# First group of a fused kernel: W2's pieces rounded one pair of matmuls later, pieces and decays dealt out anew between GpSimd and VectorE, first tile evicted by VectorE

## The reference

```python
for t in range(S):                                   # linear attention with decay w
    cur = einsum('bhd,bhe->bhde', u * kt, vt)
    y[:, :, t] = einsum('bhd,bhde->bhe', rt, state + cur)
    state = w * state + einsum('bhd,bhe->bhde', kt, vt)
x = y as rows of 384
xn = (x - mean) / sqrt(var + 1e-6) * g_ln            # channel mixing
x = x + relu(xn @ w_ch1) @ w_ch2                     # 384 -> 1536 -> 384
e = expert of the token (argmax of logits, or the one before, by a gate)
out = p[e] * (relu(x @ w1[e]) @ w2[e])               # 384 -> 1024 -> 384, 8 experts
```

## Time and profile before

| | us |
|---|---|
| time, median of 3 runs (lowest to highest) | 398.2 (398.12 to 398.61) |
| the profiled execution's own time | 399.55 |
| its span | 397.7 |
| PE busy | 382.9 (96%) |
| DVE busy | 229.1 (58%) |
| ACT busy | 161.8 (41%) |
| POOL busy | 121.8 (31%) |
| DMA moved | 54.90 MB, mean 138 GB/s |

### The profile page before, as it was taken

The page is one execution under the profiler, slowest core; times in us unless marked ns, Lnnn a source line. Parts: engine busy times, 40 slices in busy tenths (PEclk is TensorE's granted clock), DMA queues, the critical chain, the costliest instruction groups (busy, mean ns, idle before and its releaser), DMA issues.

```text
span 397.7 us, 8980 instructions
## 1 busy us (share of the span) xinstructions
PE 382.9 (96%) x3173; PEld 348.2 (88%) x3173; DVE 229.1 (58%) x463; ACT 161.8 (41%) x300; POOL 121.8 (31%) x112
## 2 busy tenths in 40 slices
PE   8796999999999999999999999999999999999993
PEld 6686999999999999999999955689999999999983
DVE  7867954622633462254376947888854665629351
ACT  5636223232322323232244145376745672555530
POOL 2893190650362054000000400622332233223232
PEclk9997999999999999999999999999999999999999
DMA  7995300520330042310105578399893559201111
GB/s 214 325 328 151 107 21 23 159 75 20 105 106 20 20 154 77 131 50 2 39 3 203 175 213 284 106 348 320 297 370 124 186 139 369 76 31 42 28 40 45
DMA packets 32633, 54.90 MB, mean 138 GB/s; under 512 B 3261, under 2 KB 20323, under 8 KB 32592
## 3 DMA queue, kind: packets, MB, share of 16 engines
q1 hardware_dynamic: 30288, 48.07, 37.1%
q0 software_dynamic: 2304, 6.30, 5.3%
HBM read 49.64 MB, written 5.51 MB: 139 GB/s over the span
## 4 chain that ended last, share of the span: by engine, by line
PE 91%; DMA 2%; ACT 2%; DVE 1%; issue 1%; SPq 1%; POOLq 0%; DVEq 0%
PE bank L1000 7%; PE bank L894 6%; PE bank L896 6%; PE bank L895 6%; PE bank L1002 6%; PE bank L1006 6%; PE bank L1299 5%; PE bank L1307 5%; PE bank L1271 5%; PE bank L1303 5%; PE bank L1278 5%; PE bank L1275 5%; PE bank L1288 3%; PE bank L909 3%; PE bank L1200 3%; PE bank L1177 3%
## 5 line engine op out<-in xcount | busy, mean ns | idle before, releaser
L687 ACT ACTIVATE parts<-bank 128x512 fp32r<-128x512 f32 x36 | 21.5, 596 | 75.6 <-PE bank L1006 75.6
L1462 DVE SCALAR_TENSOR_TENSOR parts<-bank,parts 128x512 fp32r<-128x512 f32 x36 | 24.9, 692 | 47.4 <-ACT parts L687 47.3
L630 POOL DMA_INDIRECT out_y<-late x14 | 20.5, 1462 | 93.7 <-DVE late L1805 93.7
L894 PE MATMUL bank<-parts 128*128 128x384 f32 x144 | 49.0, 341 | 0.0
L896 PE MATMUL bank<-parts 128*128 128x384 f32 x144 | 48.2, 335 | 0.0
L895 PE MATMUL bank<-parts 128*128 128x384 f32 x144 | 48.1, 334 | 0.0
L770 ACT ACTIVATE parts<-stage (+1 forms) x32 | 46.2, 1486 | 2.3 <-DMA stage<-in_w 2.2
L1000 PE MATMUL bank<-xnT_hi,parts 128*128 128x256 f32 x216 | 41.5, 301 | 3.2 <-DVE parts L1421 3.2
L1774 DVE TENSOR_TENSOR parts<-stage,parts x24 | 41.1, 1755 | 5.2 <-ACT parts L770 4.5
L1006 PE MATMUL bank<-xnT_lo,parts 128*128 128x256 f32 x216 | 38.2, 286 | 0.0
L1002 PE MATMUL bank<-xnT_hi,parts 128*128 128x256 f32 x216 | 38.2, 286 | 0.0
(11 more groups left out here) (245 smaller groups left out, 763.1 us busy)
## 6 DMA issues: line engine op xcount, KB each, us to landing
stage<-in_w SPq DMA_DIRECT2D x36, 768.0 KB, 7.8
stage<-in_w_ch SPq DMA_DIRECT2D x6, 768.0 KB, 10.1
arena<-in_k_t SPq DMA_DIRECT2D x12, 224.0 KB, 3.9
arena<-in_r_t SPq DMA_DIRECT2D x12, 224.0 KB, 3.1
arena<-in_v_rows SPq DMA_DIRECT2D x12, 192.0 KB, 4.2
arena<-in_k_rows SPq DMA_DIRECT2D x12, 192.0 KB, 3.6
x_rows<-stage SPq DMA_DIRECT2D x12, 192.0 KB, 1.9
arena<-in_r_rows SPq DMA_DIRECT2D x10, 192.0 KB, 3.3
```

What stands on the lines that cost most here:

```text
L687: act.activation(hT_hi[:, 2 * q:2 * q + 2, :].rearrange("p a t -> p (a t)"), bk[6 + q % 2][:], ACT.Relu).then_inc(h_hi_ready, 1)
L894: pe.matmul(out_, a_lo, b_hi, start=start, stop=False)
L1462: dve.scalar_tensor_tensor(hT_lo[:, at, :].rearrange("p a t -> p (a t)"), bk[6 + q % 2][:], 0.0, hT_hi[:, at, :].rearrange("p a t -> p (a ...
```

## The change

It touches the start and the first group only; nothing is added to or taken from the later groups and the experts.

- **ScalarE** rounds piece 3 behind pair 2's eviction (before: behind pair 1's), piece 4 behind pair 3's and the decay (before: behind pair 2's), piece 5 behind pair 4's. It rounds piece 0 in two halves, with the centring of the two tiles between them, it evicts only the second tile's transpose, and it makes `w_chunk` (before: VectorE).
- **VectorE** evicts the first tile's transpose alone (`first_turned`: hi, then lo), does the decays of chunk 2 (`third_decays`), masks half of chunk 0's scores before the decays of chunk 1, and `coefs(2)` behind `masked(2)`. It no longer makes lo of pieces 1 and 4, nor the product `rkT[1]`.
- **GpSimd** takes over these: `second_products`, lo of piece 1 behind both halves of piece 0, and lo of piece 4 behind `diagonal(3)`, once VectorE has made lo of pieces 2 and 3. It drops the decays of chunk 2.
- **TensorE** has ten small matmuls without use more (`keep_warm(5)`) ahead of the first transpose. Pair 2 waits for `lo_p` 3 (GpSimd's piece 1), step f = 4 for `lo_p` 4 (GpSimd's piece 4).
- **SP** issues piece 5 behind `lo_p` 3 (before: behind `lo_v` 1).

The diff, cut to its core:

```diff
-LO_V = 1, 2, 3, 4, 5
+LO_V = 2, 3, 5
@@ SP, piece(i)
                     if i == 4:
                         sp.wait_ge(lo_p, 2)
                     else:
-                        sp.wait_ge(lo_v, LO_V.index(i - 4) + 1)
+                        sp.wait_ge(lo_p, 3)
@@ GpSimd
+            def second_products():
+                pool.wait_ge(kdec_ready, 2)
+                pool.wait_ge(rdec_ready, 2)
+                pool.tensor_tensor(rkT[1], kT[1], rT[1], ALU.mult).then_inc(rkT_ready, 1)
+
+            def rest_of_piece(i):
+                pool.wait_ge(hi_done, i + 2)
+                pool.tensor_tensor(piece_at(i, 1), piece_stage(i), piece_at(i, 0).bitcast(F32),
+                                   ALU.subtract).then_inc(lo_p, 1)
...
             k_decays(1)
+            second_products()
             diagonal(0)
...
+            diagonal(1)
             ends(0)
-            diagonal(1)
             first_piece(0)
             ends(1)
             first_piece(1)
-            for c in (2, 3):
-                decays(c)
-                if c == 2:
-                    pool.wait_ge(lo_v, 1)
-                    pool.wait_ge(s_u, 16)
-                rows(c)
-                ends(c)
+            pool.wait_ge(kdec_ready, 3)
+            rest_of_piece(1)
+            pool.wait_ge(s_u, 16)
+            rows(2)
+            ends(2)
+            diagonal(2)
+            decays(3)
+            rows(3)
+            ends(3)
+            diagonal(3)
+            pool.wait_ge(lo_v, 2)
+            rest_of_piece(4)
+            pool.wait_ge(lo_v, len(LO_V))
@@ ScalarE, group(g)
                 hidden(g, range(1, 2))
-                if first:
-                    round_piece(3)
-                else:
+                if not first:
                     logits(g - 1, 1)
                 decay(g * 2 + 2, 0)
                 hidden(g, range(2, 3))
                 if first:
-                    round_piece(4)
+                    round_piece(3)
                 hidden(g, range(3, 4))
                 decay(g * 2 + 3, 1)
                 if first:
+                    round_piece(4)
+                hidden(g, range(4, 5))
+                if first:
                     round_piece(5)
-                hidden(g, range(4, NHP))
+                hidden(g, range(5, NHP))
@@ ScalarE, start
-            round_piece(0)
-            act.wait_ge(s_ng, 1)
+            act.activation(w_chunk[:], pw[:, :, C - 1], ACT.Copy).then_inc(s_wc, 1)
+            round_first(0)
             for u in range(2):
                 centre_tile(0, u)
-            for u in range(2):
-                turned_tile(0, u)
+            round_first(1)
+            act.wait_ge(s_ng, 1)
+            turned_tile(0, 1)
             round_piece(1)
@@ TensorE, hidden
-                        if q < 2:
+                        if q < 3:
                             pe.wait_ge(lo_p, q + 1)
-                        elif q % 2 == 0:
-                            pe.wait_ge(lo_v, LO_V.index(q // 2) + 1)
+                        elif q == 4:
+                            pe.wait_ge(lo_v, LO_V.index(2) + 1)
@@ TensorE, rows_out
-                        pe.wait_ge(lo_v, LO_V.index(KD + f // 4) + 1)
+                        pe.wait_ge(*((lo_p, 4) if f == 4 else (lo_v, LO_V.index(KD + f // 4) + 1)))
@@ TensorE, start
+            keep_warm(5)
             pe.wait_ge(coef_ready, 2)
             turn_tile(0, 0)
@@ VectorE
+            def third_decays():
+                dve.wait_ge(s_turned[0], T_FIRST[0] + T_LOADS)
+                dve.tensor_tensor(rT[0], rT[0], w_r, ALU.mult).then_inc(rdec_ready, 1)
+                dve.tensor_tensor(kT[0], kT[0], w_k, ALU.mult).then_inc(kdec_ready, 1)
...
-            dve.tensor_copy(w_chunk[:], pw[:, :, C - 1]).then_inc(s_scan, 1)
-            dve.wait_ge(s_ng, 1)
-            turned(0)
-            rest_of_piece(1)
+            first_turned()
+            turned(0, range(1, 2))
+            third_decays()
```

More of the change, by code:

```diff
@@ L556, in diagonal @@
                                    coef[u][:].unsqueeze(2).to_broadcast([P, H, D]), ALU.mult).then_inc(cv_ready, 1)
+            def second_products():
[6 more added lines that the diff above has]
+                                   ALU.subtract).then_inc(lo_p, 1)
             def first_piece(half):
-                pool.wait_ge(hi_done, 1)
+                pool.wait_ge(hi_done, half + 1)
                 at = slice(half * GT, (half + 1) * GT)
@@ L579, in _ @@
             first_piece(1)
-            for c in (2, 3):
-                decays(c)
-                if c == 2:
-                    pool.wait_ge(lo_v, 1)
-                    pool.wait_ge(s_u, 16)
-                rows(c)
-                ends(c)
+            pool.wait_ge(kdec_ready, 3)
[11 more added lines that the diff above has]
+            pool.wait_ge(lo_v, len(LO_V))
             for g in range(NG - 1):
-                diagonal(2 * g + 2)
-                diagonal(2 * g + 3)
-                if g == 0:
-                    pool.wait_ge(lo_v, len(LO_V))
+                if g >= 1:
+                    diagonal(2 * g + 2)
+                    diagonal(2 * g + 3)
                 for c in (2 * g + 4, 2 * g + 5):
@@ L650, in decay, with round_first @@
                 i.then_inc(decayed_ready, 1)
+            def round_first(half):
+                act.wait_ge(s_piece[0], 16)
+                at = slice(half * GT, (half + 1) * GT)
+                act.activation(piece_at(0, 0)[:, :, at], piece_stage(0)[:, :, at], ACT.Copy).then_inc(hi_done, 1)
             def round_piece(i):
@@ L756, in _ @@
             deviation(0)
+            act.wait_ge(s_wc, 1)
             group(0)
@@ L1369, in second_decays, with first_products @@
                 dve.tensor_tensor(rT[1], rT[1], w_r, ALU.mult).then_inc(rdec_ready, 2)
[L1371 to L1374 removed]
+            def first_products():
+                dve.wait_ge(kdec_ready, 1)
+                dve.wait_ge(s_pair, NP_)
+                dve.tensor_tensor(rkT[0], kT[0], rT[0], ALU.mult).then_inc(rkT_ready, 1)
+            def third_decays():
+                dve.wait_ge(s_turned[0], T_FIRST[0] + T_LOADS)
+                dve.tensor_tensor(rT[0], rT[0], w_r, ALU.mult).then_inc(rdec_ready, 1)
+                dve.tensor_tensor(kT[0], kT[0], w_k, ALU.mult).then_inc(kdec_ready, 1)
             def first_coefs(c, bank):
@@ L1386, in coefs, with masked @@
                                   ALU.add).then_inc(coef_ready, 1)
-            def masked(c, banks, sc):
-                for half in range(2):
+            def masked(c, banks, sc, halves=range(2)):
+                for half in halves:
                     dve.wait_ge(score_mm, c * 2 + half + 1)
@@ L1447, in scales, with first_turned, turned @@
                 ln_step(g, LN_STEPS, dve.tensor_tensor(rstd[:, two], rstd0[:, two], sq[:, two], ALU.mult))
-            def turned(g):
-                for u in range(2):
+            def first_turned():
+                dve.wait_ge(s_ng, 1)
+                dve.wait_ge(xnT_mm, 1)
+                for k in range(KD):
+                    i = dve.tensor_scalar(xnT_hi[:, k, 0:P], bk[0][:, k * P:(k + 1) * P], ngcol[:, k:k + 1], None,
+                                          ALU.mult)
+                i.then_inc(s_hi0, 1)
+                dve.wait_ge(s_hi0, 1)
+                for k in range(KD):
+                    i = dve.scalar_tensor_tensor(xnT_lo[:, k, 0:P], bk[0][:, k * P:(k + 1) * P], ngcol[:, k:k + 1],
+                                                 xnT_hi[:, k, 0:P].bitcast(F32), ALU.mult, ALU.subtract)
+                    if k == 0:
+                        i.then_inc(xnT_hi_ready, 1)
+                i.then_inc(xnT_ready, 1)
+            def turned(g, tiles=range(2)):
+                for u in tiles:
                     dve.wait_ge(xnT_hi_ready, g * 2 + u + 1)
@@ L1532, in group @@
                 hidden(g, range(0, 1))
-                coefs(g * 2 + 2, 0)
+                if not first:
+                    coefs(g * 2 + 2, 0)
                 hidden(g, range(1, 2))
                 masked(g * 2 + 2, bk[0:2], scT[0])
+                if first:
+                    coefs(g * 2 + 2, 0)
                 hidden(g, range(2, 3))
@@ L1550, in group @@
                 rows_of(g * 2 + 3, 1, bk[4])
-                if first:
-                    rest_of_piece(4)
                 means(g + 1)
@@ L1566, in _ @@
             decays_by_pair()
-            raw_products(0)
+            first_products()
             dve.wait_ge(s_const, 16)
-            masked(0, bk[0:2], scT[0])
+            masked(0, bk[0:2], scT[0], range(1))
             second_decays()
-            raw_products(1)
+            masked(0, bk[0:2], scT[0], range(1, 2))
             first_coefs(0, bk[3])
```

10 lines of the change are left out of this document (3 added, 7 removed).

## The result

| | before | changed |
|---|---|---|
| median, us (lowest to highest, 6 runs each) | 398.36 (397.78 to 398.61) | 395.28 (394.16 to 396.07) |
| profiled execution's own time / span | 399.55 / 397.7 | 395.42 / 393.6 |

The ratio is 0.9922 (0.9903 to 0.9942): faster, by 3.1 us. The forecast was 5.0 us and 393.2.

A forecast was written before the change was run, and what follows sets the result against it. TensorE was taken as the bound (91% busy). Hole and clock 5.68 us, less 0.3, 0.35 and 0.2 for waits, gave 4.8, the lists 5.0; 5.0 off the median 398.2 gave 393.2 us, range 391.9 to 395.2.

The forecast's parts named there:

- The hole's cause: First group, ahead of pair 4: ScalarE, waiting for piece 3's DMA, delays pair 2's eviction; TensorE idles 3.25 us.
- case 3: GpSimd and VectorE hinder each other more: 128x1536 subtraction takes 4.2 us, 0.7 paid twice, 394.6 us; chance 0.12.
- The three waits: TensorE's first group: waits of 0.9 us at pair 2, 0.9 at chunk 2's gain, 0.35 at chunk 3's gain.
- case 4: Clock falls all the same, two 0.9 us waits standing 2 us apart: 2.43 us lost, 395.6 us; chance 0.07.
- the slower one: Pair 2 waits for GpSimd's piece 1, its subtraction taking 5.3 us, and the clock falls: 399.2 us; chance 0.04.
- the one with the hole moved to W2: Nothing won: hole moves to W2, 5 us at f = 4 or 8, pieces rounded later: 398.2 us; chance 0.02.
- No new waits: GpSimd's chain is faster or the start further ahead: 6.3 us won, 391.9 us; chance 0.13.
- Hole and clock 5.68: First group: 3.25 us hole ahead of pair 4 plus 2.43 us of low clock, together 5.68 us to win.
- taken off its time this is 394.55, off the median **393.2 us: End of the sum: 5.0 us gain subtracted from the profiled execution's 399.55 and from the median of 398.2.
- the price of the clock: Pair 4 and chunk 3 take 6.87 us against 4.44 at full clock: low clock costs 2.43 us.

The follow-up runs named there:

- all_but_act: Changed kernel with ScalarE's roundings of W2's pieces 3 to 5 back in their old places; 398.63 us, ratio 1.0017 to before.
- act_only: Kernel before with only ScalarE's new places for the roundings of pieces 3 to 5; 397.50 us, ratio 0.9992 to before.
- piece4_dve: Changed kernel with the lo of piece 4 given back from GpSimd to VectorE; 396.28 us, ratio 0.9947 to before.
- before_again: Kernel before, unchanged, run again for a second profile; 398.35 us, ratio 1.0009.
- late_before: Kernel before with one further load of 0.39 MB queued ahead of piece 3's; 398.88 us, ratio 1.0037 to before.
- before_warm: Kernel before with 24 small matmuls without use filling the hole ahead of pair 4; 398.26 us, ratio 1.0006 to before.
- before_third: Kernel before, unchanged, run for a third profile; 397.83 us, ratio 0.9991.

## Why the prediction was off

**Right.** The hole's cause was ScalarE's place for piece 3 (all_but_act keeps the hole, act_only loses it). The thought in case 3 that a hand-over between VectorE and GpSimd may give nothing did not hold for piece 4 (0.8 us, piece4_dve); for piece 1 no run tells. The clock stayed at 1.00. On TensorE, forecast and measured: chunk 2's gain 26.95 and 26.82, pair 4 32.5 and 32.35, W2 39.4 and 39.04, the wait at f = 4 0.2 and 0.19; GpSimd's subtraction 3.5 and 3.50; piece 1's lo 20.25 to 23.75 and 20.16 to 23.66; piece 2's lo 28.85 to 31.9 and 28.95 to 31.56. VectorE did wait out GpSimd's second decay. The three waits were sized too large: 0.9 ahead of pair 2 is 0.37 (the scores start at 22.27 and are over at 23.4), 0.9 ahead of the gain is 0.64 (pair 2 takes 2.4 us, not 2.2), and the 0.35 ahead of chunk 3's gain did not come, GpSimd's second ends being through at 34.5 and not at 34.9. Of the rivals, the blocking of case 3, the clock of case 4, the slower one and the one with the hole moved to W2 did not happen. "No new waits" (391.9) did not either.

**The step that failed** is the sum: "Hole and clock 5.68", and "taken off its time this is 394.55, off the median **393.2 us**". A gain read from one execution was taken off the median of others, as if the 1.35 us between them stood elsewhere. The runs put them, in good part, into the very term. In that execution piece 3 landed at 29.18 and the clock was low for 6.83 us; with an earlier landing and 3.41 us the last block was already at 384.93 to 385.79 (before_again, late_before), and from there to 382.0 are 2.9 to 3.8 us, not 5.0. Off the profiled execution's own time the forecast was 394.55 for a measured 395.42; these 0.87 us are the tail, 1.10 longer, less the 0.22 by which TensorE did better than 5.0. The 2.1 us by which 393.2 missed 395.28 are in sum 1.35 + 1.10 - 0.22 - 0.14. That the tail stays as it was, the prediction assumed without naming it. The lost microseconds were thus ones that the kernel before pays only sometimes; the change takes these too, and with them most of the spread: 395.65 to 401.79 in one set of 35 executions before, 393.89 to 396.07 in 18 of the changed kernel.

**The second part of it** is the price of the clock. 6.87 - 4.44 = 2.43 us is right for that execution, but with the short stretch it is 1.5 (8.14 less 6.65). And in the kernel before it is worth less than it lasts, as VectorE's lo's of pieces 4 and 5 are next late there (before_warm: 0.85 us given back in W2's first tile). In the changed kernel they are late by 0.19 alone, GpSimd having taken one (piece4_dve: 0.8 us), so that nearly the whole stretch is won.

**Open.** What decides between 3.41 and 6.83 us isn't shown: the hole was 2.31 us in all_but_act, 2.72 in before_again and 3.34 in late_before with the short stretch, 3.25 and 3.93 with the long one, so its length alone doesn't. In the two profiles with the long stretch the clock had fallen 1.2 and 1.9 us before pair 4 started (34.27 in the first profile, 34.23 in before_third); in the three with the short one it fell between 0.1 us before that start (34.00, before_again) and 1.1 us behind it (36.01, late_before; 35.45, 0.85 behind, in all_but_act). What that order has to do with the length is not shown. Nor is it shown what the single moves of the change are worth, piece 4's hand-over and the small matmuls apart. And how often each kernel meets the longer tail is known only as far as the clusters go; the profiles of both have shown it. No version tried beats the changed kernel.

## What to carry to other kernels

Before a stall is priced from one profile, hold that execution's time and mean clock against those of the other runs: where it is above the median, the stall, above all one that hangs on a DMA's landing and brings the clock down, may be just what is larger in it, and the gain is then to be taken off its own time. Price such a stall by what is next late once it is gone. And where an engine is late, look whether it worked or waited: ahead of the masks of act_only VectorE had waited 2.73 us for one GpSimd instruction that stood too far down in its list. An eviction that stands behind the wait for a transfer wanted only later lets that transfer's landing into the time; here mending this order showed in the median and in the spread only together with the other lists (act_only alone: 0.9992).
